# Gated attention, mixture of experts and a max-of-three layer: buffer clearing, weight prefetch and first token tiles in another order

## Chip, core and metric

The kernel is one program on one core of a Trainium2 chip. A core has five engines with instruction streams of their own, which meet only through semaphores: TensorE (PE in the profile, with its weight loads as PEld), VectorE (DVE), ScalarE (ACT), GpSimd (POOL) and SyncE (SP, which here only issues DMAs and waits). The metric is the time of one execution on the device in microseconds (us); lower is better. The time before is 1131.16 us, the median of three runs (1129.34 to 1133.46).

## What is computed

Three layers follow one another. The first is a gated linear attention with complex decay, the second sends each of its 3072 output rows through the one of 8 experts that a gate chooses, and the third is a dense layer. Cut to the two that the change touches or feeds:

```python
x = attn_out.transpose(0, 2, 1, 3).reshape(3072, 384)

# experts: D = 384, E = 8, F = 1024
logits = x @ w_gate
e_idx = argmax(logits, axis=1)
gate_w = softmax(logits)[arange(N), e_idx]
eom = sigmoid(x @ w_output_gate)
for e in range(8):
    mask = e_idx == e
    h = maximum(x[mask] @ w1[e], 0)
    out[mask] = gate_w[mask, None] * eom[mask, e, None] * (h @ w2[e])

# last layer: 384 -> 768 -> 384
h = maximum(maximum(x @ w1, x @ w2), x @ w3)
return h @ w_out
```

All tensors are float32 in DRAM.

## The kernel before

**Three stages.** `attention` writes its rows to a DRAM scratch tensor `y_dram` and keeps the gate logits in `lg`. `experts` follows, then `last_layer`. At the border of two stages the engines meet in a barrier, since buffers of one stage lie where those of the next will be. The change is wholly in `experts`, which begins at about 481 us of the profile and ends at about 812 us.

**Planning.** The 3072 tokens are sorted by expert. VectorE works out each token's expert, weight and place (L1050 to L1082), with two small matmuls for the counts. Then it makes two kinds of matrices for the sort: `sent` (L1086), which holds token number, weight and expert spread over the 24 tiles of the sorted order, and `at_row` (L1088), a one-hot matrix of the row within a tile. Both are made in four parts, by turns, each part for 6 of the 24 token tiles. TensorE multiplies them (L1164, 24 matmuls into one bank, a pair of waits ahead of each 6). VectorE reads the sum out as `token` (L1090, integers) and `saux` (L1091), and goes on to the plan of visits (L1094 to L1106): 31 visits, each one a tile of 128 sorted rows with one expert. The last write of `plan` raises `planned`.

**Gathers.** GpSimd fetches the sorted rows from `y_dram` with 24 indirect DMAs (L990), one per tile, into a ring of four buffers `xs`. The first four wait only for `token`; from the fifth on each waits until TensorE has transposed the buffer's old content (`xT_ok`). Between the fourth and the fifth gather GpSimd clears `acc` (L987), the buffer of 128 x 9216 floats into which VectorE adds each visit's result. GpSimd runs its stream in order.

**Weights.** SyncE issues the loads of experts 0 and 1 at the start of the stage (L958, L959). It then waits for `planned`, for each of the two experts' loads (and raises `expert_in` after each), for the first two gathers, and issues the four loads of the last layer's weights (L972, the `prefetch` list into `raw` buffers, which are read only after 812 us). After that it loads experts 2 to 7, each when the visits that use its slot's old content are done.

**TensorE** fills idle time in the planning with matmuls whose result nobody reads (`fill`), transposes tile 0 (`tile_in(0, 6)`, L1169), waits for `planned`, reads the tile and expert numbers of the first visit into registers (L1180, L1181) and runs `up(0)`: 24 float32 matmul instructions, 48 records in the profile. It then transposes tile 1, runs `up(1)` and `down(0)`, and from there alternates `up(v+1)` and `down(v)`. Each `up` transposes one further tile (L1187) ahead of its products, until all are in.

**ScalarE** copies the transposed tiles from PSUM to SBUF (`tile_out`, L1003), the first two ahead of the wait for `planned`; then per visit it makes the upper halves of the hidden rows (L1011) and of the second weights (L1023). **VectorE** makes the lower halves (L1115, L1123) and adds the visit's result into `acc` (L1137); ahead of the first addition it waits for the clearing.

Of the kernel before, what the change touches and what calls it, by code (L numbers as in the profile page):

```python
# [21 lines left out]
ALU = mybir.AluOpType  # L22
# [3 lines left out]
P = 128  # L26
# [18 lines left out]
NT = N // P  # L45
# [859 lines left out]
def experts(nc, moe_w1, moe_w2, y_dram, lg, cmat, cvec, acc, token, prefetch):  # L905
    ctx = ExitStack()
    with ctx:
        def sb(name, shape, dt=F32):
            return ctx.enter_context(nc.sbuf_tensor(name, shape, dt))
# [4 lines left out]
        def sem(name):  # L914
            return ctx.enter_context(nc.semaphore(name))
# [7 lines left out]
        in_col = sb("in_col", [P, NT, NT])  # L923
        sent = sb("sent", [P, NT, 3, NT])
        off = sb("off", [P, E])
        offs = sb("offs", [P, E])
        aux = sb("aux", [P, NT, 3])
# [7 lines left out]
        NX = 4  # L935
# [12 lines left out]
        s = {n: sem(n) for n in names}  # L948
        w_in = [s["w_in0"], s["w_in1"]]
        gathered = [s[f"gathered{n}"] for n in range(NX)]  # L950
# [6 lines left out]
        def load_expert(sp, e):  # L957
            sp.dma_start(W1[:, e % 2].rearrange("p (c f) -> p c f", c=KD), moe_w1[e].rearrange("(c p) f -> p c f", p=P)).then_inc(w_in[e % 2], 16)  # L958
            sp.dma_start(W2[:, e % 2].rearrange("p (c d) -> p c d", c=KF), moe_w2[e].rearrange("(c p) d -> p c d", p=P)).then_inc(w_in[e % 2], 16)  # L959

        @block.sync
        def _(sp):
            for e in range(2):
                load_expert(sp, e)
            sp.wait_ge(s["planned"], 1)
            for e in range(2):
                sp.wait_ge(w_in[e], 32)
                sp.sem_inc(s["expert_in"], 1)
            for n in range(2):
                sp.wait_ge(gathered[n], 16)  # L970
            for dst, src in prefetch:
                sp.dma_start(dst, src).then_inc(s["wl_in"], 16)  # L972
            for e in range(E - 2):

                before = sp.value_load(plan[0:1, 2, e:e + 1], min_val=1, max_val=VISITS)
                sp.wait_ge(s["down_ok"], before)
                load_expert(sp, e + 2)
                sp.wait_ge(w_in[e % 2], 32 * (e // 2 + 2))
                sp.sem_inc(s["expert_in"], 1)
            sp.wait_ge(s["wl_in"], len(prefetch) * 16)  # L980

        @block.gpsimd
        def _(pool):
            pool.wait_ge(s["tokens_ok"], 1)
            for n in range(NT):
                if n == NX:
                    nc.gpsimd.memset(acc[:], 0.0).then_inc(s["acc_zero"], 1)  # L987
                if n >= NX:
                    pool.wait_ge(s["xT_ok"], n - NX + 1)
                pool.indirect_dma_start(out=xs[:, n % NX, :], out_offset=None, in_=y_dram,  # L990
                                        in_offset=bass.IndirectOffsetOnAxis(ap=token[:, n:n + 1], axis=0),
                                        bounds_check=N - 1, oob_is_err=False).then_inc(gathered[n % NX], 16)
# [43 lines left out]
        def _(dve):  # L1036
            made = [0]

            def link(ins):

                made[0] += 1
                ins.then_inc(s["decided"], 1)
                dve.wait_ge(s["decided"], made[0])

            def over(x, n):
                return x.unsqueeze(2).broadcast_to([P, x.shape[1], n])
# [33 lines left out]
            link(nc.vector.tensor_scalar(slot_a[:], slot_a[:], ROUND, ROUND, ALU.add, ALU.subtract))  # L1080
            link(nc.vector.scalar_tensor_tensor(out=slot_b[:], in0=slot_a[:], scalar=-float(P), in1=slot_f[:], op0=ALU.mult, op1=ALU.add))
            link(nc.vector.tensor_tensor(in_col[:], cvec[:, 128:128 + NT].unsqueeze(1).broadcast_to([P, NT, NT]), over(slot_a[:], NT), ALU.is_equal))  # L1082
            for part in range(4):
                own = slice(part * NT // 4, (part + 1) * NT // 4)
                shape = [P, NT // 4, 3, NT]
                nc.vector.tensor_tensor(sent[:, own], in_col[:, own].unsqueeze(2).broadcast_to(shape), aux[:, own].unsqueeze(3).broadcast_to(shape), ALU.mult).then_inc(s["sent_ok"], 1)  # L1086
                iota = cvec[:, 128:256].unsqueeze(1).broadcast_to([P, NT // 4, P])
                nc.vector.tensor_tensor(at_row[:, own], iota, over(slot_b[:, own], P), ALU.is_equal).then_inc(s["rows_ok"], 1)  # L1088
            dve.wait_ge(s["sorted_ok"], 1)
# [16 lines left out]
            nc.vector.tensor_copy(plan[:, 2, 0:E - 1], at_exp[:]).then_inc(s["planned"], 1)  # L1106
            dve.wait_ge(s["saux_ok"], 1)
            dve.wait_ge(s["planned"], 1)

            def hidden_low(v):  # L1110
                p = v % 2
                for half in range(2):
                    at = slice(half * 512, (half + 1) * 512)
                    dve.wait_ge(s["hid_high_ok"], v * 2 + half + 1)
                    nc.vector.scalar_tensor_tensor(out=hid_l[:, p, at], in0=banks[2 * p + half][:], scalar=0.0, in1=hid_h[:, p, at],  # L1115
                                                   op0=ALU.max, op1=ALU.subtract).then_inc(s["hid_low_ok"], 1)
# [8 lines left out]
            def add(v):  # L1125
                tile = dve.value_load(plan[0:1, 0, bass.ds(v, 1)], min_val=0, max_val=NT - 1)
                if not isinstance(v, int) or v >= 1:
                    dve.wait_ge(s["added"], v)

                nc.vector.scalar_tensor_tensor(out=wm[:, 0:1], in0=saux[:, 2, bass.ds(tile, 1)], scalar=v_exp[:, bass.ds(v, 1)],  # L1130
                                               in1=saux[:, 1, bass.ds(tile, 1)], op0=ALU.is_equal, op1=ALU.mult).then_inc(s["weigh_ok"], 1)
                dve.wait_ge(s["down_ok"], v + 1)
                dve.wait_ge(s["weigh_ok"], v + 1)
                if isinstance(v, int) and v == 0:
                    dve.wait_ge(s["acc_zero"], 1)
                a = acc[:, bass.ds(tile * DM, DM)]
                nc.vector.scalar_tensor_tensor(out=a, in0=banks[4 + v % 2][:, 0:DM], scalar=wm[:, 0:1], in1=a, op0=ALU.mult, op1=ALU.add).then_inc(s["added"], 1)  # L1137

            for v in range(VISITS):
                hidden_low(v)  # L1140
                weights_low(v, range(GW2 // 2))
                if v:
                    add(v - 1)
                weights_low(v, range(GW2 // 2, GW2))
            add(VISITS - 1)

        @block.tensor
        def _(pe):
            def fill(count):
                for _ in range(count):  # L1150
                    nc.tensor.matmul(banks[3][:, 0:3 * P], cmat[:, 2, :], cmat[:].rearrange("p m c -> p (m c)"), start=True, stop=True)
# [5 lines left out]
            nc.tensor.matmul(banks[1][:, 0:NT * E], cmat[:, 2, :], picks, start=True, stop=True).then_inc(s["ranked"], 1)  # L1157

            fill(11)
            for n in range(NT):  # L1160
                if n % (NT // 4) == 0:
                    pe.wait_ge(s["sent_ok"], n // (NT // 4) + 1)
                    pe.wait_ge(s["rows_ok"], n // (NT // 4) + 1)
                ins = nc.tensor.matmul(banks[2][:, 0:3 * NT], at_row[:, n], sent[:, n].rearrange("p c n -> p (c n)"), start=(n == 0), stop=(n == NT - 1))  # L1164
            ins.then_inc(s["sorted_ok"], 1)

            def tile_in(n, bk):
                for c in range(KD):
                    ins = nc.tensor.transpose(banks[bk][:, c * P:(c + 1) * P], xs[:, n % NX, c * P:(c + 1) * P], ident)  # L1169
                ins.then_inc(s["xT_ok"], 1)  # L1170

            fill(7)
            pe.wait_ge(gathered[0], 16)
            tile_in(0, 6)
            pe.wait_ge(s["planned"], 1)
            pe.wait_ge(s["saux_ok"], 1)

# [45 lines left out]
                ins.then_inc(s["down_ok"], 1)  # L1223

            up(0, 0, None, 0)
            pe.wait_ge(gathered[1], 16)
            tile_in(1, 7)
            up(1, 1, 2, 2)
            down(0, 0)
            up(2, 0, 3, 3)  # L1230
# [227 lines left out]
```

## Time and profile before

| what | value |
|---|---|
| three runs | 1133.46, 1129.34, 1131.16 us; median 1131.16 |
| the profiled execution | 1133.46 us, with a span of 1131.7 us |
| TensorE matmul busy | 1018.7 us (90% of the span) |
| VectorE, ScalarE, GpSimd busy | 643.9, 564.0, 212.8 us |
| mean granted clock of TensorE | 0.905 of full speed |

The span runs from the first to the last instruction that the profile shows; the execution's own time is 1.8 us longer. The profiled execution is the slowest of the three. TensorE is busy for most of the span in all stages. Its clock is granted at one of two levels, 1.0 (2.4 GHz) and 0.5 (1.2 GHz). Of the stage borders the one at 481 us matters here: between the last matmul of the attention and the first product of the experts lies the planning, in which TensorE's work is mostly filling.

### The profile page before, as it was taken

To read this page: it belongs to the slowest core of one execution; us is meant where nothing else is said; L and a number is where in the kernel's file an instruction comes from. 1 tells how busy PE (TensorE), PEld (TensorE's weight loads), DVE (VectorE), ACT (ScalarE), POOL (GpSimd) and SP (SyncE) were. 2 spreads that over 40 slices of the span, in tenths; PEclk is the share of its full clock that TensorE was granted. 3 is DMA by queue.
4 is the path that set the end of the run, shared out by engine and by line. 5 is a ranking of instruction groups with operands and counts; after the bars stand their busy time and mean duration, and the time that the engine had idled before them with its cause. 6 is when DMAs were issued, how large, how long until landed. Compare 5 with 4: busy or idle time off the path is not lost. (4 is left out here: it accounts for less than half of the span.)

```text
span 1131.7 us, 27378 instructions
## 1 busy us (share of the span) xinstructions
PE 1018.7 (90%) x10480; PEld 875.1 (77%) x10481; DVE 643.9 (57%) x1373; ACT 564.0 (50%) x910; POOL 212.8 (19%) x193
## 2 busy tenths in 40 slices
PE   5768877878788779889999999999899999999997
PEld 3556656666566657669999999999788888888886
DVE  5587878888888877665555565666641212121210
ACT  7677767777777676205554445544532222222221
POOL 2221212122213122032101110000012222222222
PEclk9677787887787878789999999999999999999999
DMA  9331434242524121084330323130000000000000
GB/s 185 74 78 37 100 65 86 51 99 51 113 49 88 39 56 42 24 292 162 128 132 21 133 87 106 58 112 0 0 1 29 1 28 1 28 8 22 17 12 28
DMA packets 172050, 74.86 MB, mean 66 GB/s; under 512 B 152864, under 2 KB 165280, under 8 KB 171936
## 3 DMA queue, kind: packets, MB, share of 16 engines
q1 hardware_dynamic: 165408, 59.15, 20.9%
q0 software_dynamic: 3072, 9.44, 2.5%
q10 hardware_dynamic: 3456, 4.72, 1.1%
q8 instruction: 75, 1.23, 0.5%
q14 instruction: 39, 0.32, 0.1%
HBM read 63.86 MB, written 9.44 MB: 65 GB/s over the span
## 5 line engine op out<-in xcount | busy, mean ns | idle before, releaser
L1201 PE MATMUL B<-xT,W 128*128 x1488 | 173.0, 277 | 2.4 <-issue 2.3
L1201 PEld LDWEIGHTS B<-xT,W 128*128 128x128 f32 x1488 | 170.7, 193 | 2.9 <-issue 2.9
L1123 DVE TENSOR_TENSOR W2l<-W,W2h 128x768 fp32r<-128x768 f32 x124 | 113.3, 955 | 36.9 <-ACT W2h L1023 36.0
L1388 PE MATMUL L<-zT,high 128*128 128x512 f32 x324 | 127.1, 392 | 2.0 <-ACT high L1307 2.0
L1388 PE MATMUL L<-zT,low 128*128 128x512 f32 x324 | 126.9, 392 | 0.0
L1388 PE MATMUL L<-zT_low,high 128*128 128x512 f32 x324 | 126.8, 392 | 0.0
L1023 ACT ACTIVATE W2h<-W 128x768 fp32r x124 | 104.6, 847 | 33.9 <-PE B L1219 31.6
L303 POOL TENSOR_TENSOR qn<-qe,trig 128x384 f32<-128x384 f32 x48 | 64.8, 1350 | 246.3 <-ACT trig L375 232.4
L1290 POOL TENSOR_TENSOR h_low<-h_full,hz 128x512 fp32r<-128x512 f32 x36 | 46.4, 1289 | 316.6 <-ACT hz L1325 316.6
L1360 DVE TENSOR_TENSOR m<-L,m 128x512 f32<-128x512 f32 x36 | 24.9, 691 | 132.3 <-PE L L1388 132.3
L1325 ACT ACTIVATE hz<-h_full 128x512 fp32r<-128x512 f32 x36 | 22.7, 632 | 150.8 <-DVE h_full L1366 150.8
L1011 ACT ACTIVATE hid_h<-B 128x512 fp32r<-128x512 f32 x62 | 36.9, 598 | 111.6 <-PE B L1201 111.6
L1115 DVE SCALAR_TENSOR_TENSOR hid_l<-B,hid_h 128x512 fp32r<-128x512 f32 x62 | 42.8, 692 | 84.4 <-ACT hid_h L1011 84.4
L805 PE MATMUL KV<-vblk,k3n 64*96 64x96 f32 x768 | 56.8, 299 | 34.5 <-DVE state L652 34.2
L1219 PE MATMUL B<-W2h,hid_h 128*128 128x384 f32 x248 | 85.8, 346 | 0.1
L805 PEld LDWEIGHTS KV<-vblk,k3n 64*96 64x96 f32 x768 | 48.2, 201 | 48.7 <-issue 48.5
L643 DVE TENSOR_TENSOR T<-M,fac 96x192 f32<-96x192 f32 x192 | 83.3, 434 | 2.4
L1219 PE MATMUL B<-W2l,hid_h 128*128 128x384 f32 x248 | 83.6, 337 | 0.0
L1219 PE MATMUL B<-W2h,hid_l 128*128 128x384 f32 x248 | 83.3, 336 | 0.0
L1388 PEld LDWEIGHTS L<-zT,high 128*128 128x128 f32 x324 | 61.4, 189 | 15.0 <-issue 2.4
L1388 PEld LDWEIGHTS L<-zT_low,high 128*128 128x128 f32 x324 | 61.4, 189 | 12.7
L1388 PEld LDWEIGHTS L<-zT,low 128*128 128x128 f32 x324 | 61.2, 189 | 12.8
(179 smaller groups left out, 2053.7 us busy)
## 6 DMA issues: line engine op xcount, KB each, us to landing
W<-in_moe_w SPq DMA_DIRECT2D x16, 1536.0 KB
are<-in_a_re SPq DMA_DIRECT2D x12, 384.0 KB, 3.9
aim<-in_a_im SPq DMA_DIRECT2D x12, 384.0 KB, 5.1
qin<-in_q SPq DMA_DIRECT2D x24, 192.0 KB, 3.1
kin<-in_k SPq DMA_DIRECT2D x24, 192.0 KB, 3.4
vin<-in_v SPq DMA_DIRECT2D x24, 192.0 KB, 3.3
vblk<-in_v SPq DMA_DIRECT2D x96, 48.0 KB, 2.4
attention_rows<-ysb ACTq DMA_DIRECT2D x24, 192.0 KB, 3.2
```

The costliest lines, as they stand in the source:

```text
L303: nc.gpsimd.tensor_tensor(qn[:, p], x, trig[:, h:h + GH], ALU.mult).then_inc(s["q_nat"], 1)
L643: nc.vector.tensor_tensor(T[:, j % 2], M[:, g % 2, j], carried(g, CHUNKS + 1 + j), ALU.mult).then_inc(s["t_ok"], 1)
L805: ins = nc.tensor.matmul(KV[a][0:C2, h * 2 * D:(h + 1) * 2 * D], k3n[at, p, h].rearrange("p c d -> p (c d)"), vblk[at, gg * GH + h].rearra ...
L1011: nc.scalar.activation(hid_h[:, p, half * 512:(half + 1) * 512], banks[2 * p + half][:], ACT.Relu).then_inc(s["hid_high_ok"], 1)
L1023: nc.scalar.activation(W2h[:, g], w2raw[:, bass.ds(base + g * GC, GC)], ACT.Copy).then_inc(s["w2_high_ok"], 1)
L1115: nc.vector.scalar_tensor_tensor(out=hid_l[:, p, at], in0=banks[2 * p + half][:], scalar=0.0, in1=hid_h[:, p, at], op0=ALU.max, op1=ALU.su ...
L1123: nc.vector.tensor_tensor(W2l[:, g], w2raw[:, bass.ds(base + g * GC, GC)], W2h[:, g], ALU.subtract).then_inc(s["w2_low_ok"], 1)
L1201: ins = nc.tensor.matmul(banks[2 * p + half][:, j % 4 * P:(j % 4 + 1) * P], W1[:, w, c * FF + j * P:c * FF + (j + 1) * P], xf[:, bass.ds(x ...
L1219: ins = nc.tensor.matmul(banks[4 + p][:, 0:DM], h_[:, p, j * P:(j + 1) * P], w_[:, g, at:at + DM], start=(j == 0 and k == 0), stop=(j == K ...
L1290: nc.gpsimd.tensor_tensor(h_low[:, j], h_full[:, u % 2], hz[:, j], ALU.subtract).then_inc(s["h_low"], 1)
L1360: nc.vector.tensor_tensor(m2[:], banks[1 + 3 * (u % 2)][:], m1[:], ALU.max).then_inc(s["m2_ok"], 1)
L1388: ins = nc.tensor.matmul(out_, stationary(a_, c), moving(b_, c), start=(c == 0 and k == 0), stop=(c == count - 1 and k == 2))
```

## The change

It has four parts, all in `experts`.

1. SyncE issues the four `prefetch` loads right behind the loads of experts 0 and 1. Its waits for the first two gathers are gone.
2. GpSimd clears `acc` ahead of all gathers, as soon as the last part of `at_row` is made (`rows_ok` at 4). VectorE waits for the clearing at the end of the planning and no longer at the first addition.
3. `sent` is made by one VectorE instruction, ahead of the four parts of `at_row`.
4. TensorE transposes tile 1 together with tile 0, ahead of its wait for `planned`.

```diff
--- before.py
+++ after.py
@@ -962,14 +962,12 @@
         def _(sp):
             for e in range(2):
                 load_expert(sp, e)
+            for dst, src in prefetch:
+                sp.dma_start(dst, src).then_inc(s["wl_in"], 16)
             sp.wait_ge(s["planned"], 1)
             for e in range(2):
                 sp.wait_ge(w_in[e], 32)
                 sp.sem_inc(s["expert_in"], 1)
-            for n in range(2):
-                sp.wait_ge(gathered[n], 16)
-            for dst, src in prefetch:
-                sp.dma_start(dst, src).then_inc(s["wl_in"], 16)
             for e in range(E - 2):
 
                 before = sp.value_load(plan[0:1, 2, e:e + 1], min_val=1, max_val=VISITS)
@@ -981,10 +979,10 @@
 
         @block.gpsimd
         def _(pool):
+            pool.wait_ge(s["rows_ok"], 4)
+            nc.gpsimd.memset(acc[:], 0.0).then_inc(s["acc_zero"], 1)
             pool.wait_ge(s["tokens_ok"], 1)
             for n in range(NT):
-                if n == NX:
-                    nc.gpsimd.memset(acc[:], 0.0).then_inc(s["acc_zero"], 1)
                 if n >= NX:
                     pool.wait_ge(s["xT_ok"], n - NX + 1)
                 pool.indirect_dma_start(out=xs[:, n % NX, :], out_offset=None, in_=y_dram,
@@ -1080,10 +1078,9 @@
             link(nc.vector.tensor_scalar(slot_a[:], slot_a[:], ROUND, ROUND, ALU.add, ALU.subtract))
             link(nc.vector.scalar_tensor_tensor(out=slot_b[:], in0=slot_a[:], scalar=-float(P), in1=slot_f[:], op0=ALU.mult, op1=ALU.add))
             link(nc.vector.tensor_tensor(in_col[:], cvec[:, 128:128 + NT].unsqueeze(1).broadcast_to([P, NT, NT]), over(slot_a[:], NT), ALU.is_equal))
+            nc.vector.tensor_tensor(sent[:], in_col[:].unsqueeze(2).broadcast_to([P, NT, 3, NT]), aux[:].unsqueeze(3).broadcast_to([P, NT, 3, NT]), ALU.mult).then_inc(s["sent_ok"], 1)
             for part in range(4):
                 own = slice(part * NT // 4, (part + 1) * NT // 4)
-                shape = [P, NT // 4, 3, NT]
-                nc.vector.tensor_tensor(sent[:, own], in_col[:, own].unsqueeze(2).broadcast_to(shape), aux[:, own].unsqueeze(3).broadcast_to(shape), ALU.mult).then_inc(s["sent_ok"], 1)
                 iota = cvec[:, 128:256].unsqueeze(1).broadcast_to([P, NT // 4, P])
                 nc.vector.tensor_tensor(at_row[:, own], iota, over(slot_b[:, own], P), ALU.is_equal).then_inc(s["rows_ok"], 1)
             dve.wait_ge(s["sorted_ok"], 1)
@@ -1106,6 +1103,7 @@
             nc.vector.tensor_copy(plan[:, 2, 0:E - 1], at_exp[:]).then_inc(s["planned"], 1)
             dve.wait_ge(s["saux_ok"], 1)
             dve.wait_ge(s["planned"], 1)
+            dve.wait_ge(s["acc_zero"], 1)
 
             def hidden_low(v):
                 p = v % 2
@@ -1131,8 +1129,6 @@
                                                in1=saux[:, 1, bass.ds(tile, 1)], op0=ALU.is_equal, op1=ALU.mult).then_inc(s["weigh_ok"], 1)
                 dve.wait_ge(s["down_ok"], v + 1)
                 dve.wait_ge(s["weigh_ok"], v + 1)
-                if isinstance(v, int) and v == 0:
-                    dve.wait_ge(s["acc_zero"], 1)
                 a = acc[:, bass.ds(tile * DM, DM)]
                 nc.vector.scalar_tensor_tensor(out=a, in0=banks[4 + v % 2][:, 0:DM], scalar=wm[:, 0:1], in1=a, op0=ALU.mult, op1=ALU.add).then_inc(s["added"], 1)
 
@@ -1157,9 +1153,9 @@
             nc.tensor.matmul(banks[1][:, 0:NT * E], cmat[:, 2, :], picks, start=True, stop=True).then_inc(s["ranked"], 1)
 
             fill(11)
+            pe.wait_ge(s["sent_ok"], 1)
             for n in range(NT):
                 if n % (NT // 4) == 0:
-                    pe.wait_ge(s["sent_ok"], n // (NT // 4) + 1)
                     pe.wait_ge(s["rows_ok"], n // (NT // 4) + 1)
                 ins = nc.tensor.matmul(banks[2][:, 0:3 * NT], at_row[:, n], sent[:, n].rearrange("p c n -> p (c n)"), start=(n == 0), stop=(n == NT - 1))
             ins.then_inc(s["sorted_ok"], 1)
@@ -1170,8 +1166,9 @@
                 ins.then_inc(s["xT_ok"], 1)
 
             fill(7)
-            pe.wait_ge(gathered[0], 16)
-            tile_in(0, 6)
+            for n in range(2):
+                pe.wait_ge(gathered[n], 16)
+                tile_in(n, 6 + n)
             pe.wait_ge(s["planned"], 1)
             pe.wait_ge(s["saux_ok"], 1)
 
@@ -1223,8 +1220,6 @@
                 ins.then_inc(s["down_ok"], 1)
 
             up(0, 0, None, 0)
-            pe.wait_ge(gathered[1], 16)
-            tile_in(1, 7)
             up(1, 1, 2, 2)
             down(0, 0)
             up(2, 0, 3, 3)
```

The rows of the changed program below carry its own line numbers, which are a few lower. First GpSimd's stream at the start of the stage; `acc` is the cleared buffer, `xs` the ring of gathered rows. Before:

```order
L982 UNCONDITIONAL_BRANCH [waits barrier_Pool_Activation_PE_DVE_SP_gather]
L990 DMA xs<-attention_rows,token 128x384 [waits tokens_ok]
L990 DMA xs<-attention_rows,token 128x384 x3
L987 MEMSET acc 128x9216
L990 DMA xs<-attention_rows,token 128x384 [waits xT_ok] x20
L907 UNCONDITIONAL_BRANCH
```

and now:

```order
L980 UNCONDITIONAL_BRANCH [waits barrier_Pool_Activation_PE_DVE_SP_gather]
L983 MEMSET acc 128x9216 [waits rows_ok]
L988 DMA xs<-attention_rows,token 128x384 [waits tokens_ok]
L988 DMA xs<-attention_rows,token 128x384 x3
L988 DMA xs<-attention_rows,token 128x384 [waits xT_ok] x20
```

The clearing has moved ahead of the four gathers that it followed.

Now TensorE's stream from the last filling matmuls on; `xs` transposed by `cmat` is a token tile, `plan` the table of visits. Before, tile 1's transposes stand 24 matmuls further down, behind `up(0)`:

```order
L1151 MATMUL B<-cmat 128x384 x7
L1169 MATMUL B<-cmat,xs 128x128 [waits gathered0]
L1169 MATMUL B<-cmat,xs 128x128 x2
L1180 TENSOR_LOAD plan [waits saux_ok,planned]
L1180 ISA x2
L1181 TENSOR_LOAD plan
L1181 ISA x2
L1189 REGISTER_ALU
L1190 REGISTER_ALU [waits expert_in]
L1205 REGISTER_ALU [waits xT_out]
```

and now:

```order
L1147 MATMUL B<-cmat 128x384 x7
L1165 MATMUL B<-cmat,xs 128x128 [waits gathered0]
L1165 MATMUL B<-cmat,xs 128x128 x2
L1165 MATMUL B<-cmat,xs 128x128 [waits gathered1]
L1165 MATMUL B<-cmat,xs 128x128 x2
L1177 TENSOR_LOAD plan [waits saux_ok,planned]
L1177 ISA x2
L1178 TENSOR_LOAD plan
L1178 ISA x2
L1186 REGISTER_ALU
L1187 REGISTER_ALU [waits expert_in]
L1202 REGISTER_ALU [waits xT_out]
```

The three transposes of tile 1, with the wait for the second gather, stand ahead of the register loads of the first visit.

Last, SyncE's stream; `W` are the experts' weights, `raw` those of the last layer. Before:

```order
L958 DMA W<-in_moe_w 128x3x1024
L959 DMA W<-in_moe_w 128x8x384
L958 DMA W<-in_moe_w 128x3x1024
L959 DMA W<-in_moe_w 128x8x384
L972 DMA raw<-in_moe_w 128x3x768 [waits planned,w_in0,w_in1,gathered1,gathered0]
L972 DMA raw<-in_moe_w 128x3x768 x2
L972 DMA raw<-in_moe_w_out 128x6x384
L975 TENSOR_LOAD plan
L975 ISA x2
```

and now:

```order
L958 DMA W<-in_moe_w 128x3x1024
L959 DMA W<-in_moe_w 128x8x384
L958 DMA W<-in_moe_w 128x3x1024
L959 DMA W<-in_moe_w 128x8x384
L966 DMA raw<-in_moe_w 128x3x768 x3
L966 DMA raw<-in_moe_w_out 128x6x384
L973 TENSOR_LOAD plan [waits planned,w_in0,w_in1]
L973 ISA x2
```

The four `raw` loads have lost all their waits and directly follow the experts' loads.

## Rows read from the trace of the kernel before

**Rows 1.** Waits of PE after 504 us: who for whom, total us, times, longest
```profile
PE B L1201 <- issue: 2.3, 1, 2.3
...
PE B L1187 <- ACT xT L1003: 0.7, 1, 0.7
```

**Rows 2.** Windows: busy time (instructions) per engine, TensorE clock, DMA share, GB/s
```profile
519.90:811.70 291.80, 291.67 (x2198) 290.64 (x2198) 173.18 (x240) 144.75 (x200) 16.96 (x17) 1.00 0.22 77
```

**Rows 3.** Timeline of GpSimd: start, duration, engine, line, operation [idle before <- releaser]
```profile
499.24 1.20 POOL L990 DMA_INDIRECT xs<-attention_rows,token  x1 [44.86 <-DVE token L1090]
...
504.50 7.79 POOL L987 MEMSET acc<- 128x9216 f32 x1
512.46 1.00 POOL L990 DMA_INDIRECT xs<-attention_rows,token  x1 [0.16 <-issue]
513.77 1.00 POOL L990 DMA_INDIRECT xs<-attention_rows,token  x1 [0.30 <-issue]
```

**Rows 4.** Timeline of VectorE, 490 to 503 us
```profile
490.45 0.61 DVE L1086 TENSOR_TENSOR sent<-in_col,aux 128x432 f32<-128x432 f32 x1
490.98 0.95 DVE L1088 TENSOR_TENSOR at_row<-cvec,slot_b 128x768 f32<-128x768 f32 x1
...
495.14 0.95 DVE L1088 TENSOR_TENSOR at_row<-cvec,slot_b 128x768 f32<-128x768 f32 x1
498.15 0.18 DVE L1090 CAST token<-B 128x24 int32<-128x24 f32 x1 [2.05 <-PE B L1164]
...
502.95 0.26 DVE L1106 CAST plan<-at_exp 128x7 int32<-128x7 f32 x1
```

**Rows 5.** Timeline of TensorE, 492 to 515 us
```profile
492.63 5.47 PE L1164 MATMUL B<-sent,at_row 128*128 128x72 f32 x48
497.95 4.73 PE L1151 MATMUL B<-cmat 128*128 128x384 f32 x14
502.51 0.55 PE L1169 MATMUL B<-cmat,xs 128*128 128x128 f32 x3
505.40 7.25 PE L1201 MATMUL B<-xT,W 128*128 x48 [2.34 <-issue]
512.49 0.49 PE L1169 MATMUL B<-cmat,xs 128*128 128x128 f32 x3
513.65 0.52 PE L1187 MATMUL B<-cmat,xs 128*128 128x128 f32 x3 [0.67 <-ACT xT L1003]
514.26 0.93 PE L1201 MATMUL B<-xT,W 128*128 x6
```

**Rows 6.** The gathers issued at 502.13, 503.50 and 515.07 us: issue to landing
```profile
DMA to landing us min/median/max: 3.2/3.2/3.2
...
DMA to landing us min/median/max: 5.4/5.4/5.4
...
DMA to landing us min/median/max: 6.2/6.2/6.2
```

**Rows 7.** DMA issues of SyncE's queue, 481 to 506 us
```profile
481.86 0.48 SPq L959 DMA_DIRECT2D W<-in_moe_w  x1
...
483.00 3.23 SPq L959 DMA_DIRECT2D W<-in_moe_w  x1
503.96 1.43 SPq L972 DMA_DIRECT2D raw<-in_moe_w  x3
```

**Rows 8.** Windows, columns as in Rows 2: the two times of dense transfers
```profile
482.00:500.00 18.00, 18.00 (x85) 13.14 (x84) 14.73 (x46) 1.29 (x3) 0.76 (x1) 0.90 0.98 350
504.00:520.00 16.00, 13.83 (x104) 13.40 (x105) 5.46 (x7) 5.34 (x10) 11.29 (x5) 0.89 0.97 353
```

**Rows 9.** DMA issues by line: three of the last layer's weight loads, KB each
```profile
raw<-in_moe_w SPq DMA_DIRECT2D x3, 1152.0 KB
```

**Rows 10.** Windows, columns as in Rows 2: TensorE's granted clock
```profile
481.40:485.20 3.80, 3.73 (x8) 2.56 (x9) 3.40 (x12) 1.87 (x3) 0.00 (x0) 0.50 0.72 193
506.20:509.40 3.20, 3.20 (x17) 3.20 (x16) 0.00 (x0) 0.00 (x0) 3.20 (x1) 0.50 0.99 385
```

## The prediction

> **What bounds the kernel now.** I read the waits of TensorE first, then windows over the expert stage, then the timeline of the stretch that the change touches, engine by engine. From the first product of the experts on, TensorE waits only twice in that stage: 2.3 us ahead of `up(0)` and 0.7 us ahead of the transposes in `up(1)` [rows 1]. Between 519.9 and 811.7 us it is busy for 291.67 of 291.80 us [rows 2]. So the stage has no slack: whatever moves the start of `up(1)` moves the end of the program by as much, and whatever does not move it is worth nothing. The change has to be judged in the 25 us between the making of `sent` and that start.
>
> The chain through this stretch: the sort's result, `token` (ends 498.33), first gather of GpSimd at 499.24, its transposes at 502.51, `planned` at 503.21, about 2.2 us of register loads, `up(0)` at 505.40, tile 1's transposes at 512.49, `up(1)` at 514.26 [rows 3 to 5]. The clearing of `acc` takes 7.79 us on GpSimd and today stands behind the first four gathers. Nobody is late for it, as the next gathers feed tiles 4 and later. The reader should see in rows 3 that the gather behind it starts 0.16 us after its end, though the buffer it needed was free since 503.06: GpSimd does one thing at a time.
>
> **Part 1, one `sent`.** A VectorE product of 432 elements takes 0.61 us and one of 768 takes 0.95 us [rows 4]: 1.03 us per 1000 elements. 1728 elements in one piece are then 0.6 + 1.34 = 1.94 us. Starts of neighbours lie 0.07 to 0.08 us closer than the durations say, so the first `at_row` starts at 490.45 + 1.87 = 492.32 and ends at 493.27, against 491.93 before; the fourth ends at 492.32 + 3 x 0.87 + 0.95 = 495.88, against 496.09. The sort on TensorE is 48 records in 5.47 us without a gap [rows 5], so it is limited by itself and starts 1.3 us later: `token` ends at about 499.6 instead of 498.3, `planned` comes at about 504.5. By itself this would cost 1.3 us. Behind part 2 it is hidden, since the gathers will not start before 504.
>
> **Part 2, the clearing first.** It starts when the fourth `at_row` is done, 495.9 plus 0.1 us for the semaphore, and takes 7.79 us: end at 503.8. The first gather follows after 0.16 us, at 503.95, instead of 499.24; the second 1.31 us later (512.46 to 513.77 in rows 3), at 505.3. VectorE's new wait for the clearing stands behind the plan, which ends at 504.5 by part 1. Queued behind it is only the first lower half of the hidden rows, for which VectorE waits much longer anyway. Cost nothing; without that cover it would be under a microsecond.
>
> How long does a gather take to land? The one issued at 502.13 needed 3.2 us, the ones issued at 503.50 and 515.07, in the company of the `raw` loads, 5.4 and 6.2 us [rows 6]. Which of these holds depends on part 3.
>
> **Part 3, the prefetch early.** The fourth expert load held SyncE's queue for 3.23 us where the second took 0.48 us, so the queue pushes back when much is outstanding [rows 7]. The experts' 6.3 MB move at 350 GB/s from 482 to 500 us [rows 8]. The four `raw` loads, of 1152 KB each [rows 9] (the fourth has as many elements), will now follow without a gap: 4.7 MB plus the gathers' 0.4 MB at 353 to 390 GB/s, the rate of the second dense window and somewhat above, fill the DMA engines from 499 to about 512.5 us. Pushed back again, SyncE comes free when most of the experts' data have landed, about 497 us, and at worst at 499; `expert_in` is wanted after 511. Nothing lost there. But both first gathers now lie wholly in the dense time, where before they had idle engines. I take 6.2 us for each, the row of the gather that lay wholly inside it; the bounds are 3.2 and 6.4 us (3.2 is the idle price). Tile 1 lands at 505.3 + 6.2 = 511.5.
>
> The Trainium skill ("DMA: Bandwidth & Descriptors", section "Queues, rings and completion order") says that each DMA engine takes the queues that have work by turns and finishes a whole packet of one before it switches. So a small gather waits its turn behind packets of the weight queue; by that rule the dense price holds for both gathers, and by the opposite view (the gather passes at once) the idle one. The three rows agree with the rule.
>
> **Part 4, tile 1 ahead of `planned`.** This makes the second gather, not the first, the thing that `up(0)` waits for. Its transposes start at 511.6. Before, `planned` at 503.21 led to `up(0)` at 505.40, 2.19 us of register loads; from the transposes of tile 0 to `up(0)` it was 2.89 us [rows 5]. Now the loads stand behind the transposes of tile 1: between 2.2 and 2.9 us, I take 2.5. `up(0)` starts at 514.1, **8.7 us later** than before.
>
> What it gives back: tile 1's transposes and the wait for ScalarE's copy between `up(0)` and `up(1)` go. Before, 512.49 to 514.26 are 1.77 us; now only the transposes of tile 2 and the step to the products stand there, 513.65 to 514.26 = 0.61 us, and their gather (issued near 506.6, landed by 513) is in time. That is 1.1 us gained. ScalarE and VectorE can start visit 0 while `up(0)` runs, instead of after 513; TensorE did not wait for them before, so this is worth nothing.
>
> The clock: in `up(0)` it was granted at half for 3.2 us after the short pause before it [rows 10]. TensorE now idles from about 504 (the end of the filling, shifted by 1.3 us) to 514 but for six transposes, so `up(0)` will start at the lower level. When it did so at 481.4, the level stayed for 3.8 us of steady work [rows 10]. 0.6 us more at the low level cost some 0.3 us; bounds 0 and 1.6 us (half of the 3.2 us at the half clock, once more). I take 0.1, since the count may start with the transposes.
>
> **Sum:** 8.7 - 1.1 + 0.1 = **+7.7 us** at the start of `up(1)`, and so at the end. On the profiled execution, 1133.46 us, that gives 1141.2. That one is the slowest of three and 2.3 us above their median, so against the median 1131.16 I forecast **1138.9 us**, 0.7% slower.
>
> **Rivals.**
>
> *The gathers land as if alone (3.2 us).* Then tile 1 is in at 508.5, `up(0)` starts at 511.1, and the sum is 5.7 - 1.1 + 0.1 = +4.7: 1135.9 us. For it speaks that the `raw` loads start earlier and might be thinning out; against it that 13 us of data follow 499 us. Chance 0.15.
>
> *The clearing stops VectorE.* If a writing GpSimd shuts VectorE out, `token` comes only at 503.8 + 0.2, and the first gather 0.9 us behind it (498.33 to 499.24 in rows 3 and 4), at 504.9 instead of 503.95: +8.7, or 1139.9 us; if it is the clearing that is stretched by the VectorE work beside it, each microsecond of stretch is one of the total. Before, the clearing ran with an idle VectorE, so no row decides. Chance 0.12. The Trainium skill ("SBUF — State Buffer", section "Who interferes with whom") calls the port pair that VectorE and GpSimd share an exclusive lock, taken by VectorE only in its two-port modes and for two-input operations against a reading GpSimd. A clearing only writes and `token` is read from PSUM, so by the rule only the last small casts of `plan` could be held, for which nobody hurries; no run here shows it yet.
>
> *Not slower: the gathers pass the clearing.* If GpSimd's descriptor work can start while the clearing runs, the first gather is issued 0.9 us behind `token`, at 500.5, and the second at 502.0. Landing alone in 3.2 us, tile 1 is in at 505.2, `up(0)` starts at 507.8, and the sum is 2.4 - 1.1 + 0.1 = +1.4: 1132.6 us. With the dense price it is +4.4. The point from which it decides: for a sum within 3.4 us tile 1 must have landed by 507.2. Against it stands the gather that waited for the end of the clearing with its buffer free for 9 us [rows 3]. Chance 0.05, and 0.03 more for any gain in a stage that I have not seen.
>
> *The order has no effect*, because the loads do not really start earlier: then part 3 falls away and it is the first rival's number.
>
> **How the numbers follow.** The forecast has 0.65, the stopped VectorE 0.12, the lone gathers 0.15, the other side 0.08. The likeliest case alone: landing 5.4 instead of 6.2 and 2.2 instead of 2.5 us take 1.1 off, the clock's upper bound adds 1.5, and the median of three wanders by a microsecond or two: 1136.5 to 1142.5. The range over the cases takes in most of the lone gathers: 1134.5 to 1143. What a measurement of this kernel can tell from no change is about 0.3%, 3.4 us. Both slower cases lie above it and the lone gathers (+4.7) a little above, so I put slower at 0.85, within 0.3% at 0.12, faster at 0.03.
>
> **What would show it.** In the changed profile: the clearing at 496, 7.8 us long; the first gather right behind it near 504; the second landing near 511.5; TensorE idle for some 7 us between filling and transposes, put down to a DMA; `up(0)` near 514 at half clock; `up(1)` 7.9 us behind the start of `up(0)` instead of 8.9; no wait from there to the end of the stage, with the end moved by as much. I am wrong if the gathers start before the clearing ends, if they land in 3.2 us, if the clearing is much longer or shorter than 7.8 us, or if TensorE shows idle time after `up(1)` that soaks up the shift.

## The result and the profile after

The changed kernel is slower: 1140.13 us median of 4 runs (1137.99 to 1141.91) against 1130.49 us (1129.34 to 1133.46). The ratio is 1.007, 95% interval 1.0049 to 1.0092, which on 1130.5 us is +7.9 us (5.5 to 10.4). Forecast were +7.7 us and 1138.9 us. The two medians of four lie 9.6 us apart, which is more than the ratio says; over all 16 executions of the changed kernel on record the median is 1138.7 us.

The profiled execution has a span of 1137.1 us. The attention stage, which the change does not touch, ends at a different moment in each execution: over all profiles of this study the first expert load is issued between 476.5 and 483.3 us. So I count every time below from that issue (481.43 us in the profile before, 479.18 after) and write it as "at 23.97". TensorE's waits from 500 us on:

```profile
PE B L1165 <- DMA xs<-attention_rows,token: 6.9, 2, 6.5
...
PE B L1198 <- ACT xT L1001: 1.4, 1, 1.4
```

The 2.3 us and the 0.7 us of [rows 1] are gone; in their place stand 6.9 us for gathered rows and 1.4 us ahead of `up(0)`. The profile puts the 1.4 us down to ScalarE's copy of tile 1, but that copy ended at 510.52 us, 0.8 us before `up(0)`; what ended last are the register loads (L1177, L1178), which run from 509.2 to about 511.1 us. Why the gathered rows come late, GpSimd's timeline shows (columns as in [rows 3]):

```profile
493.70 7.78 POOL L983 MEMSET acc<- 128x9216 f32 x1 [38.79 <-DVE at_row L1085]
501.65 1.20 POOL L988 DMA_INDIRECT xs<-attention_rows,token  x1 [0.17 <-issue]
503.16 1.01 POOL L988 DMA_INDIRECT xs<-attention_rows,token  x1 [0.31 <-issue]
```

The clearing takes as long as before and starts as soon as `at_row` is made; the gathers follow behind it, at 22.47 and 23.98 instead of 17.81 and 19.32 [rows 3]. `token` had been ready at 17.77. TensorE, to be held against [rows 5]:

```profile
491.18 5.55 PE L1160 MATMUL B<-sent,at_row 128*128 128x72 f32 x48 [0.60 <-DVE at_row L1085]
496.57 4.73 PE L1147 MATMUL B<-cmat 128*128 128x384 f32 x14
507.81 0.90 PE L1165 MATMUL B<-cmat,xs 128*128 128x128 f32 x3 [6.51 <-DMA xs<-attention_rows,token]
509.10 0.90 PE L1165 MATMUL B<-cmat,xs 128*128 128x128 f32 x3 [0.38 <-DMA xs<-attention_rows,token]
511.35 8.57 PE L1198 MATMUL B<-xT,W 128*128 x48 [1.36 <-ACT xT L1001]
519.76 0.49 PE L1184 MATMUL B<-cmat,xs 128*128 128x128 f32 x3
520.29 3.94 PE L1198 MATMUL B<-xT,W 128*128 x33
```

Both groups of transposes and most of `up(0)` run slowly, 0.90 instead of 0.55 us and 8.57 instead of 7.25 us. VectorE, against [rows 4]:

```profile
488.21 1.96 DVE L1081 TENSOR_TENSOR sent<-in_col,aux 128x1728 f32<-128x1728 f32 x1
490.09 3.56 DVE L1085 TENSOR_TENSOR at_row<-cvec,slot_b 128x768 f32<-128x768 f32 x4
...
496.77 0.18 DVE L1087 CAST token<-B 128x24 int32<-128x24 f32 x1 [3.13 <-PE B L1160]
```

And SyncE's queue, against [rows 7]:

```profile
484.02 9.24 SPq L966 DMA_DIRECT2D raw<-in_moe_w  x3
493.30 2.23 SPq L966 DMA_DIRECT2D raw<-in_moe_w_out  x1
```

The prefetch is issued early, and pushed back for 11.5 us, but SyncE is free at 16.35, well before `planned`. What that early issue does to the DMA engines, and the wait to the clock, the windows show (columns as in [rows 2]):

```profile
499.00:504.00 5.00, 2.29 (x8) 1.02 (x6) 2.60 (x7) 0.00 (x0) 4.53 (x3) 0.99 1.04 402
504.00:509.50 5.50, 1.31 (x5) 0.91 (x6) 0.00 (x0) 0.49 (x1) 2.17 (x4) 0.50 1.05 387
511.30:517.20 5.90, 5.85 (x27) 5.85 (x28) 0.00 (x0) 0.24 (x1) 0.48 (x1) 0.50 0.23 70
```

While the first two gathers are under way the DMA engines are full (shares 1.04 and 1.05); the clock is at 0.50 from 504 us on and stays there for the first 5.9 us of `up(0)`.

`up(1)` starts at 41.11 against 32.83, 8.3 us later. From there to the end of the span it is 616.8 us against 617.4, so 7.65 us arrive at the end; of the 0.6 us between, 0.2 are a shorter wait at the start of the last layer, and the rest I cannot place.

### The profile page after: what moved, and what is told of

Same layout as the page of the kernel before. It is cut to its first block and busy times, and to the rows that moved or that the text cites. A ratio compares the mean times of both kernels' runs of the same rounds, so it can differ in the third digit from the quotient of the medians.

```text
span 1137.1 us, 27372 instructions
## 1 busy us (share of the span) xinstructions
PE 1019.0 (90%) x10480; PEld 874.9 (77%) x10481; DVE 643.4 (57%) x1370; ACT 564.3 (50%) x910; POOL 212.1 (19%) x193
```

## Experiments

All are versions of one of the two kernels with one or a few edits. The table has the issue of the first expert load in each profile, and the profiled times from there, in us: second gather issued; the last transposes that `up(0)` waits for; `up(0)`, its duration; `up(1)`; and the ratio to the kernel before from the timed runs.

| run | load | gather | transposes | up(0) | lasts | up(1) | ratio (95%) |
|---|---|---|---|---|---|---|---|
| before | 481.43 | 19.32 | 21.08 | 23.97 | 7.25 | 32.83 | 1 |
| after | 479.18 | 23.98 | 29.92 | 32.17 | 8.57 | 41.11 | 1.0070 (1.0049 to 1.0092) |
| e1, prefetch late | 478.86 | 23.88 | 27.04 | 29.30 | 8.15 | 37.83 | 1.0041 (1.0026 to 1.0057) |
| e2, clearing behind | 477.99 | 20.13 | 26.22 | 28.48 | 6.97 | 35.75 | 1.0041 (1.0026 to 1.0055) |
| e3, clearing at start | 483.29 | 29.30 | 32.4 (both tiles) | 35.12 | 7.18 | 42.60 | 1.0074 (1.0051 to 1.0098) |
| e4, tile 1 behind | 479.07 | 23.97 | 28.63 | 30.89 | 8.09 | 40.60 | 1.0052 (1.0033 to 1.0071) |
| e5, parts 1 and 4 only | 476.53 | 20.18 | 23.36 | 25.62 | 8.46 | 34.45 | 1.0011 (0.9995 to 1.0027) |
| b2, part 3 only | 479.53 | 19.14 | 24.34 | 26.60 | 7.78 | 36.09 | 1.0037 (1.0022 to 1.0053) |
| b3, before with fillings | 479.09 | 19.39 | 21.20 | 24.07 | 5.62 | 31.31 | 0.9990 (0.9979 to 1.0001) |
| b4, the same and tile 1 | 477.99 | 18.76 | 22.92 | 23.47 | 5.62 | 29.39 | 0.9977 (0.9963 to 0.9990) |
| a5, after with fillings | 480.25 | 23.87 | 29.83 | 32.16 | 5.62 | 38.15 | 1.0049 (1.0033 to 1.0065) |
| e6, clearing in pieces | 476.85 | 20.34 | 26.41 | 28.66 | 8.51 | 37.55 | 1.0059 (1.0041 to 1.0076) |

The times in the middle columns come from one profile per version, and the split of the change into its terms rests on them. The timed runs tell less: only the intervals of e5, b3 and b4 lie wholly below that of the changed kernel, and only those of e5 and b3 include no change. The ratios of e1 and e2 are 0.0029 (3.3 us) below that of the changed kernel, near the 2.9 and 3.7 us found below, but their intervals overlap with its own.

**e1, the changed kernel with the prefetch late again.**

```diff
             for e in range(2):
                 load_expert(sp, e)
-            for dst, src in prefetch:
-                sp.dma_start(dst, src).then_inc(s["wl_in"], 16)
             sp.wait_ge(s["planned"], 1)
...
                 sp.sem_inc(s["expert_in"], 1)
+            for n in range(2):
+                sp.wait_ge(gathered[n], 16)
+            for dst, src in prefetch:
+                sp.dma_start(dst, src).then_inc(s["wl_in"], 16)
```

> The changed kernel with the four last-layer weight loads issued late again (behind planned, the experts' loads and the first two gathers). All times from the issue of the first expert load; up(1) starts there at 32.8 us before and at 41.1 us in the changed kernel. My theory: the second gather is issued at 24.0 us as in the changed kernel, but lands in 3.2 us instead of 5.9, so up(0) starts at 29.5 instead of 32.2 and up(1) at 38.0 (37.4 to 38.6 with the clock): about 3.1 us of the 8.3 are the company of the weight loads, total about 1136. Rival, the landing is slow for another reason (the cold queue, the clearing just before): landing stays near 6 us and up(1) at 41.

The second gather is issued at the same time. Its landing in e1:

```profile
DMA to landing us min/median/max: 3.1/3.1/3.1
```

The window around it in e1, columns as in [rows 2]:

```profile
499.00:504.00 5.00, 1.88 (x6) 0.76 (x4) 2.18 (x7) 0.00 (x0) 4.27 (x3) 0.93 0.13 37
```

And the landing of the same gather in the changed kernel:

```profile
DMA to landing us min/median/max: 5.9/5.9/5.9
```

DMA share 0.13 instead of 1.04, landing 3.1 instead of 5.9 us (the first gather: 3.3 instead of 6.1), `up(0)` 2.9 us and `up(1)` 3.3 us earlier; the last 0.4 us are a shorter `up(0)`. The company of the weight loads is the whole of that term.

**e2, the changed kernel with the clearing behind the first four gathers.** The edit puts the clearing and its wait back to where they stood before.

> The changed kernel with the clearing of acc behind the first four gathers again. Times from the issue of the first expert load. My theory: the gathers follow token (17.6 us) by 0.9 and 2.4 us, at 18.5 and 20.0, land in 6 us since the weight loads are in their way, tile 1 is in at 26.0, up(0) starts at 28.3 and up(1) at 37.1: about 4 us of the 8.3 are the clearing's place, total about 1135. Rival, the gathers could pass the clearing anyway: up(1) stays at 41. Rival, the weight loads do not slow them: landing 3.2, up(1) at 34.3.

```profile
496.61 1.20 POOL L988 DMA_INDIRECT xs<-attention_rows,token  x1 [42.98 <-DVE token L1087]
498.12 1.10 POOL L988 DMA_INDIRECT xs<-attention_rows,token  x1 [0.31 <-issue]
...
501.89 7.79 POOL L985 MEMSET acc<- 128x9216 f32 x1
```

The second gather is issued 3.85 us earlier (20.13 against 23.98) and its transposes start 6.1 us after that: `up(0)` is 3.7 us earlier, near the expected 3.9, `up(1)` 5.4 us. The other 1.6 us are a shorter `up(0)`, 6.97 us instead of 8.57. e6 below has the same pauses and took 8.51, so these 1.6 us are not the edit's. They are the clock, as windows show (columns as in [rows 2]). In e2, with `up(0)` from 506.47 us on:

```profile
506.50:509.00 2.50, 2.50 (x12) 2.50 (x13) 0.00 (x0) 0.00 (x0) 2.50 (x1) 0.50 1.05 375
509.50:513.50 4.00, 4.00 (x39) 4.00 (x37) 0.69 (x1) 0.62 (x2) 2.20 (x3) 1.00 0.44 124
```

and in e6, with `up(0)` from 505.51 us on:

```profile
505.50:511.50 6.00, 5.99 (x28) 6.00 (x29) 0.00 (x0) 0.39 (x1) 0.42 (x1) 0.50 0.78 277
```

In e2 the level is back at 1.00 within 3 us of the start of `up(0)`, in e6 it is still at 0.50 after 6 us.

**e3, the changed kernel with the clearing at the start of the stage.**

```diff
         def _(pool):
-            pool.wait_ge(s["rows_ok"], 4)
             nc.gpsimd.memset(acc[:], 0.0).then_inc(s["acc_zero"], 1)
```

> The changed kernel with the clearing at the very start of the stage, without a wait for at_row, so that it runs beside VectorE's planning of the first 8 us. Times from the issue of the first expert load. My theory, only the queue behind the clearing costs: sent is made at 9.0 us as before, the gathers are issued at 18.5 and 20.0 as in the run with the clearing behind, up(1) at 37.1. Rival, a clearing stops or slows VectorE: sent comes later by up to 7.8 us, and up(1) with it, or the clearing itself takes clearly more than 7.8 us.

My theory fell and the rival held. The clearing ran from 483.29 to 491.07 us. VectorE beside it:

```profile
485.67 0.35 DVE L1054 TENSOR_REDUCE chosen<-cum 128x24 f32<-128x192 f32 x1
486.05 0.35 DVE L1056 TENSOR_REDUCE total<-ex 128x24 f32<-128x192 f32 x1
486.44 4.66 DVE L1057 TENSOR_SCALAR total<-total 128x24 f32<-128x24 f32 x1
491.13 0.18 DVE L1059 SCALAR_TENSOR_TENSOR total<-chosen,total 128x24 f32<-128x24 f32 x1
```

Eight reductions and two-input operations from 483.32 on pass unhindered, the last two of them shown. Then a `tensor_scalar` of 24 elements, 0.18 us elsewhere, takes 4.66 us and ends with the clearing. The damage doubles on TensorE: its fillings run out 4.8 us before the sort can start, the clock falls, to 0.50 for the whole sort (499.5 to 509.9 us), and the sort takes 10.49 us instead of 5.5:

```profile
499.48 10.49 PE L1159 MATMUL B<-sent,at_row 128*128 128x72 f32 x48 [4.78 <-DVE at_row L1084]
```

So `token` starts at 26.7 (17.6 in the changed kernel), and what GpSimd no longer has in its queue is lost on VectorE and on the clock. The Trainium skill ("SBUF — State Buffer", section "Who interferes with whom") has this as an exclusive lock on a port pair that VectorE takes in its two-port modes, `tensor_scalar` and copies within SBUF among them, and holds or waits for through a whole instruction. The row agrees, in what was held and in what was not.

**e6, the same with the clearing in 24 pieces.**

```diff
-            nc.gpsimd.memset(acc[:], 0.0).then_inc(s["acc_zero"], 1)
+            for piece in range(NT):
+                nc.gpsimd.memset(acc[:, piece * DM:(piece + 1) * DM], 0.0).then_inc(s["acc_zero"], 1)
...
-            dve.wait_ge(s["acc_zero"], 1)
+            dve.wait_ge(s["acc_zero"], NT)
```

> The changed kernel with the clearing at the very start of the stage and cut into 24 pieces of 384 floats per partition. In one piece there it held one VectorE tensor_scalar for 4.66 us until the clearing ended. Times from the issue of the first expert load. My theory, one instruction of the one engine shuts out those of the other that need the same port for as long as it lasts: a VectorE operation is held for at most one piece, about 0.4 us, token at 17.6 to 18.5 instead of 26.7, up(1) near 36. Rival, GpSimd keeps what VectorE needs while it has instructions queued: VectorE is held to the end of the last piece as before, token near 26, up(1) at 42 or later.

```profile
480.00 0.18 DVE L1058 TENSOR_SCALAR total<-total 128x24 f32<-128x24 f32 x1
480.22 0.18 DVE L1060 SCALAR_TENSOR_TENSOR total<-chosen,total 128x24 f32<-128x24 f32 x1
480.44 0.50 DVE L1061 COPY aux<-cvec 128x24 f32<-128x24 f32 x1
```

The longest operation held is this copy, 0.50 us instead of 0.18; one piece of the clearing takes 0.42 us (0.37 us from start to start). `token` ends at 17.9 and the gathers are 0.2 us behind those of e2. The hold lasts no longer than one instruction of GpSimd. (`up(1)` at 37.55 was expected near 36; the 1.5 us are the clock in the row of e6 above, `up(0)` 8.51 us.) The timed runs do not tell this version from the changed kernel (1.0059 against 1.0070).

**e4, the changed kernel with tile 1 behind `up(0)`.** The edit puts part 4 back.

> The changed kernel with the transposes of tile 1 behind up(0) again. Times from the issue of the first expert load. My theory: up(0) starts 1.3 us earlier, near 30.9, since it waits for one gather only, and the gap of 1.8 us between up(0) and up(1) is back instead of 0.5: up(1) at 41.2, no change in total within 0.5 us. Rival, tile 1 ahead of planned is what costs: up(1) at 39.8. Rival, it is what gains: up(1) at 42.4.

`up(0)` starts 1.3 us earlier (30.89), the gap behind it is back, `up(1)` is at 40.60. The 0.5 us to the changed kernel are those by which `up(0)` is shorter (8.09 us). In these profiles part 4 costs and gains about the same; the timed runs (1.0052 against 1.0070) cannot tell a difference of 2 us from none.

**e5, the kernel before with parts 1 and 4 only.**

> The kernel before with only two of the four parts of the change, sent in one piece and tile 1 ahead of planned; the clearing and the prefetch stand where they were. Times from the issue of the first expert load. My theory: token 0.9 us later (17.6), second gather at 20.1, landed in 3.2 us at 23.3, up(0) at 25.7 instead of 24.0, the gap to up(1) 0.5 instead of 1.8: up(1) at 33.3 to 34.0 against 32.8 before. So clearing and prefetch are nearly all of the 8.3 us. Rival, these two parts carry 2 us or more: up(1) at 35 or later.

`up(1)` is 1.6 us later, at 34.45 where at most 34.0 was expected; 1.2 of the 1.6 us are a slower `up(0)`. In the timed runs there is no clear difference (1.0011). Clearing and prefetch carry 6.7 of the 8.3 us. At the start of `up(0)`, ahead of the clock's part, the three add up: 3.7 us come with the clearing's place (e2), 2.9 with the prefetch (e1), 1.65 with parts 1 and 4 (25.62 less 23.97), together 8.2, as measured (32.17 less 23.97). That they meet so closely is partly luck: in the four profiles with the old planning (before, b2, b3, b4) the sort starts at 11.20, 11.03, 11.28 and 10.64, so a term taken across two profiles is good to some tenths of a microsecond.

**b2, the kernel before with the early prefetch only.**

> The kernel before with only the prefetch issued early. Times from the issue of the first expert load. My theory, the first gather (17.8) now lies among the weight loads: lands in 6 us at 23.8 instead of 3.2, its transposes at 23.9, up(0) at 26.2 instead of 24.0, up(1) at 35.0 (34.7 to 36.0 by the clock): 2 to 3 us slower in total. Rival, the first gather is as quick as before because the experts' loads were still running then too: no change, 32.8.

The first gather's transposes start 6.7 us after its issue (17.64 to 24.34) instead of 3.3, `up(1)` is 3.3 us later, at 36.09, just above the expected 34.7 to 36.0. The timed runs agree that it is slower, by 4.2 us (2.5 to 6.0). The early prefetch is harmful alone too; whether it would be harmless with no gather near, no run shows.

**b3, the kernel before with three more fillings.**

```diff
             tile_in(0, 6)
+            fill(3)
             pe.wait_ge(s["planned"], 1)
```

> The kernel before with three more filling matmuls behind the transposes of tile 0, where TensorE waits 2.3 us for registers; nothing else differs. Times from the issue of the first expert load. My theory, that pause is what lowers the clock in up(0): up(0) starts at 24.0 as before, takes 5.6 us at the full clock instead of 7.25, up(1) at 31.2 instead of 32.8, 1.6 us faster in total (0.14%). Rival, the clock falls anyway: no change. Rival, the fillings delay up(0): slower by up to 0.7 us.

```profile
500.29 0.55 PE L1169 MATMUL B<-cmat,xs 128*128 128x128 f32 x3
500.68 2.10 PE L1151 MATMUL B<-cmat 128*128 128x384 f32 x6
...
503.16 5.62 PE L1202 MATMUL B<-xT,W 128*128 x48 [0.39 <-issue]
```

The fillings lie under the register loads, `up(0)` takes 5.62 us, and its start has not moved (24.07). `up(1)` gains 1.5 us in the profile; the timed runs cannot tell it from nothing.

**b4, b3 with tile 1 transposed just ahead of the first visit's products.**

```diff
+                if isinstance(v, int) and v == 0:
+                    pe.wait_ge(gathered[1], 16)
+                    tile_in(1, 7)
                 pe.wait_ge(s["expert_in"], ex_ + 1)
...
             up(0, 0, None, 0)
-            pe.wait_ge(gathered[1], 16)
-            tile_in(1, 7)
```

> As the run with three more filling matmuls on the kernel before, and the transposes of tile 1 stand behind the register loads of the first visit, just ahead of its products, instead of behind up(0). Times from the issue of the first expert load. My theory: tile 1 has landed at 22.5, so its transposes cost 0.5 us ahead of up(0) (24.5) and save the 1.8 us gap down to 0.5: up(1) at 30.6, 2.2 us faster than before (0.2%). Rival, the wait for ScalarE's copies moves ahead of up(0): no gain over the fillings alone, 31.2 or later.

```profile
498.58 0.55 PE L1169 MATMUL B<-cmat,xs 128*128 128x128 f32 x3
498.97 2.10 PE L1151 MATMUL B<-cmat 128*128 128x384 f32 x6
500.91 0.49 PE L1169 MATMUL B<-cmat,xs 128*128 128x128 f32 x3
501.46 5.62 PE L1205 MATMUL B<-xT,W 128*128 x48
506.92 0.49 PE L1188 MATMUL B<-cmat,xs 128*128 128x128 f32 x3
```

TensorE has no gap left from the fillings to `up(1)`. `up(1)` starts at 29.39; 0.6 us of the gain is an earlier `token` in this execution (16.16 against 16.72), the rest, 2.9 us, is the edit (2.2 were expected). The timed runs give 0.9977 (0.9963 to 0.9990): this version beats the kernel before by 1 to 4 us, and so the changed kernel by more (0.9977 against 1.0070).

**a5, the changed kernel with long fillings.** `fill(7)` became `fill(16)`, and `fill(3)` stands behind tile 1's transposes.

> The changed kernel with nine more filling matmuls ahead of the wait for the first gather and three behind the transposes of tile 1, so that TensorE stays busy through its two pauses. Times from the issue of the first expert load. My theory: the clock stays up, up(0) starts at 32.3 as in the changed kernel and takes 5.6 us instead of 8.6, the two groups of transposes 0.55 instead of 0.9 each; up(1) at 38.1 instead of 41.1, 3 us faster than the changed kernel and still 5 slower than before. Rival, the idle time is not what lowers the clock, or the fillings do not count: no change, 41.1.

```profile
499.52 8.55 PE L1147 MATMUL B<-cmat 128*128 128x384 f32 x26
508.68 0.55 PE L1165 MATMUL B<-cmat,xs 128*128 128x128 f32 x3 [0.61 <-DMA xs<-attention_rows,token]
510.08 0.55 PE L1165 MATMUL B<-cmat,xs 128*128 128x128 f32 x3 [0.85 <-DMA xs<-attention_rows,token]
510.46 2.10 PE L1147 MATMUL B<-cmat 128*128 128x384 f32 x6
512.41 5.62 PE L1200 MATMUL B<-xT,W 128*128 x48
```

With the same start of `up(0)` (32.16) it takes 5.62 us, and the transposes 0.55. Against the changed kernel that is 3.0 us of clock; against the kernel before, the half clock in `up(0)` had cost 1.6 us there. The timed runs (1.0049 against 1.0070) point the same way, but their intervals overlap.

## Why the prediction was right, step by step

- **Nothing behind `up(1)` has slack.** Right: no wait of TensorE from `up(1)` to the end of the stage, and the shift arrives but for 0.6 us.
- **Part 1.** `sent` took 1.96 us (1.94), the last `at_row` ended at 14.47 (14.45). The sort started 0.8 us later, not 1.3: I had it wait for `at_row` before as well, but there it stood behind the fillings, which ended at 492.8 us. Hidden, as said, behind the clearing.
- **Part 2.** Clearing at 14.52 for 7.78 us, gathers at 22.47 and 23.98; forecast were 22.52 and 23.87 (503.95 and 505.3 less 481.43). e2 returns the issue by 3.85 us. VectorE's new wait cost nothing: the clearing ended 0.26 us before the last write of `plan`.
- **Part 3.** Landing of the second gather 5.9 us (6.2), and e1 shows 3.1 without the loads. SyncE free at 16.35, so nothing lost there.
- **Part 4.** From tile 1's transposes to `up(0)` 2.25 us (I took 2.5): the register loads start with the transposes (509.2 us) and take what they took before, 2.2 us from `planned` to `up(0)`; from the first transposes behind `up(0)` to `up(1)` it is 0.53 us (519.76 to 520.29) instead of 1.77, so 1.2 us back (1.1).
- **The clock was mis-sized.** I took 0.1 us out of 0 to 1.6; measured are 1.3 us (8.57 less 7.25). The measured term lies in the bounds, but near the end that I had not chosen: the level was at half from 504 us on, with TensorE idle since the last filling ended at 501.3, and stayed there through both groups of transposes and the first 5.9 us of `up(0)`, where I had counted with 3.8 us. For the same reason a sign that I had named did not come: `up(1)` starts 8.94 us behind `up(0)`, not 7.9 (8.86 before). The 1.3 us are one pair of profiles, and not the change's alone: e5, without the new clearing and prefetch, has 1.2 us of them, and e2, with parts 1, 3 and 4, took less than the kernel before (6.97 us).
- **The total is nearer than its terms, by luck.** At `up(1)` it was 8.3 instead of 7.7 us: the clock cost 1.2 us more than forecast, the start of `up(0)` came 0.5 us earlier (8.2 instead of 8.7), and 0.1 us more was given back. Then 0.6 us, for which I had no term, were lost again behind `up(1)`, so that 7.65 us arrive where 7.7 were forecast. The two large terms, the clearing's place and the landing among the weight loads, are right by e2 and e1.

Of the rivals, the lone gathers (3.2 us) are refuted by e1 against the changed kernel, and the gathers that pass the clearing by rows of the change itself: `token` ready at 17.77, gather at 22.47. That the loads do not start earlier is refuted by SyncE's rows: the first `raw` load is issued at 4.84 (22.53 before). The stopped VectorE is real, but not in this change: under the clearing stood only reductions, two-input operations and reads from PSUM, `token` for one at its old 0.18 us; the first `tensor_scalar` of `plan` started 0.08 us before the clearing's end. e3 put the clearing over an earlier one. My 0.12 for this rival asked for a held `token`, and that did not happen.

## To carry to other kernels

Before work that "costs nothing" is moved ahead of something, look what is queued behind it on the same engine: 8 us of clearing were free behind four gathers and cost 4 in front of them. An early prefetch is not free either if small latency-bound transfers fall into its time; here the first two took 6.1 and 5.9 instead of 3.3 and 3.1 us. And where TensorE waits ahead of a stage that it bounds, cheap filling during the wait can keep its clock up (3.0 us at `up(1)` in the profile of a5, 1.5 in that of b3; in timed runs only b4, with the filling and an earlier tile 1, is clear of no change).

## What the runs showed that I had not expected

- A GpSimd clearing held a VectorE `tensor_scalar` of 24 elements for 4.66 us and let reductions and two-input operations pass (e3); in 24 pieces of 0.42 us each a copy of 0.18 us took 0.50 us (e6).
- The duration of `up(0)` after a pause is not steady: 6.97, 7.18, 7.25, 7.78, 8.09, 8.15, 8.46, 8.51 and 8.57 us in nine profiles, and 5.62 in the three whose pauses were filled (none longer than 0.85 us was left). Even e2 and e6, whose gathers and pauses are alike, differ by 1.5 us, and the length of the pauses does not order them: e5, with pauses of 0.79 and 1.71 us, took 8.46 us, e4, with 6.52 and 1.36 us, took 8.09. A term of one or two microseconds that hangs on the clock should be given as a range.
- The small casts of `plan` take 0.41, 0.33 and 0.26 us while gathers are being issued, and 0.18, 0.17 and 0.16 in e1 and in the changed kernel, where the first gather starts within 0.1 us of their end.
